# The last 384 tokens leave the sort: a plain store in place of an indirect scatter for the MLP's last step

## What is computed

```python
skip_score = x @ w_skip
do_compute = skip_score > 0
out = x.copy()
xc = x[do_compute]
e_idx = np.argmax(xc @ w_gate, axis=1)
for e in range(E):
    mask = e_idx == e
    h = np.maximum(xc[mask] @ w1[e], 0.0)
    y[mask] = gate_w[mask, None] * (h @ w2[e])
out[do_compute] = xc + y                 # skipped tokens keep x
# the MLP, on all 2304 tokens
h = out @ w_in
return np.maximum(0.01 * h, h) @ w_out
```

## Time and profile before

| | us |
|---|---|
| median of 3 runs | 777.68 |
| lowest and highest run | 777.25, 777.89 |
| the profiled execution, its own time | 777.04 |
| its span, from the first to the last instruction | 775.0 |
| TensorE matmul busy | 715.4 (92%) |
| VectorE, ScalarE, GpSimd busy | 276.1, 262.1, 183.9 |

### The profile page before, as it was taken

The page is one execution under the profiler, slowest core; times in us unless marked ns, Lnnn a source line. Parts: engine busy times, 40 slices in busy tenths (PEclk is TensorE's granted clock), DMA queues, the critical chain, the costliest instruction groups (busy, mean ns, idle before and its releaser), DMA issues.

```text
span 775.0 us, 12847 instructions
## 1 busy us (share of the span) xinstructions
PE 715.4 (92%) x4627; PEld 663.4 (86%) x4627; DVE 276.1 (36%) x577; ACT 262.1 (34%) x522; POOL 183.9 (24%) x185
## 2 busy tenths in 40 slices
PE   2989989991999999998999999999999999999994
PEld 2888878871999999997898999999998989899993
DVE  4667757757000000004323242333224333323221
ACT  4687776550111221113222222222222232223221
POOL 2120100103786667533000500230050013001001
PEclk9999999995899999999999999999999999999997
DMA  8483745788799999953000300120030012001001
GB/s 175 111 185 99 189 125 168 235 266 197 221 316 329 316 301 315 328 167 100 1 1 1 122 1 1 41 82 1 0 120 1 0 41 81 0 0 41 1 1 41
DMA packets 72920, 91.46 MB, mean 118 GB/s; under 512 B 26704, under 2 KB 47728, under 8 KB 72881
## 3 DMA queue, kind: packets, MB, share of 16 engines
q1 hardware_dynamic: 63537, 65.35, 29.5%
q0 software_dynamic: 8288, 25.57, 11.6%
q10 hardware_dynamic: 1056, 0.02, 0.1%
HBM read 73.91 MB, written 17.01 MB: 117 GB/s over the span
## 4 chain that ended last, share of the span: by engine, by line
PE 79%; SPq 6%; ACT 4%; DVE 4%; issue 3%; DMA 3%; another core or an unknown queue 2%; POOLq 0%; POOL 0%; ACTq 0%; DVEq 0%
PE psum L1568 26%; PE psum L1587 26%; PE psum L1481 9%; PE psum L1497 8%; SPq L395 4%; ACT kt L784 2%; PE psum L1321 2%; PE psum L1346 1%; DMA wg<-in_moe_w_skip_dram 1%; PE psum L1419 1%; SPq L380 1%; PE psum L1436 1%; PE psum L1507 1%; PE psum L1299 1%
## 5 line engine op out<-in xcount | busy, mean ns | idle before, releaser
L1568 PE MATMUL psum<-x2h,wih 128*128 128x384 f32 x384 | 130.6, 340 | 1.9 <-DVE x2l L1241 1.9
L1259 DVE SCALAR_TENSOR_TENSOR g_act<-g_raw 128x384 f32<-128x384 f32 x96 | 53.6, 558 | 219.3 <-ACT g_raw L947 205.5
L1568 PE MATMUL psum<-x2h,wil 128*128 128x384 f32 x384 | 129.5, 337 | 0.0
L1568 PE MATMUL psum<-x2l,wih 128*128 128x384 f32 x384 | 129.0, 336 | 0.0
L947 ACT ACTIVATE g_raw<-psum 128x384 f32<-128x384 f32 x96 | 47.2, 492 | 235.2 <-PE psum L1568 226.9
L1587 PE MATMUL psum<-woh,g_l 128*128 128x512 f32 x288 | 114.0, 396 | 0.0
L1587 PE MATMUL psum<-wol,g_h 128*128 128x512 f32 x288 | 113.7, 395 | 0.0
L1587 PE MATMUL psum<-woh,g_h 128*128 128x512 f32 x288 | 112.1, 389 | 0.7 <-DVE g_l L1263 0.7
L745 POOL DMA_INDIRECT out_dram<-o_sb,idxo x18 | 18.9, 1050 | 337.8 <-ACT o_sb L942 334.1
L1481 PE MATMUL psum<-xt,wring 128*128 128x160 f32 x512 | 81.2, 306 | 0.7 <-ACT xt L873 0.6
L1497 PE MATMUL psum<-hp,wring 128*128 128x160 f32 x512 | 77.4, 299 | 0.0
(11 more groups left out here) (173 smaller groups left out, 896.0 us busy)
## 6 DMA issues: line engine op xcount, KB each, us to landing
wring<-in_moe_w_dram SPq DMA_DIRECT2D x64, 512.0 KB, 8.5
y_rows<-zrow SPq DMA_DIRECT2D x1, 4800.0 KB
q_st<-in_q_dram SPq DMA_DIRECT2D x8, 576.0 KB
k_st<-in_k_dram SPq DMA_DIRECT2D x8, 576.0 KB
x_sb<-x_rows SPq DMA_DIRECT2D x4, 1024.0 KB, 5.9
stage<-in_moe_w_in_dram POOLq DMA_DIRECT2D x4, 1024.0 KB, 8.4
stage<-in_moe_w_out_dram POOLq DMA_DIRECT2D x4, 1024.0 KB, 9.8
vs<-in_v_dram SPq DMA_DIRECT2D x20, 128.0 KB, 7.0
```

What stands on the lines that cost most here:

```text
L1259: dve.scalar_tensor_tensor(out=g_act[:, f % 2, :], in0=g_raw[:, f % 2, :], scalar=LEAK, in1=g_raw[:, f % 2, :], op0=ALU.mult, op1=ALU.max) ...
L1568: last = pe.matmul(bank[f % 2][:, 0:MT * P], wt[:, c, f * P:(f + 1) * P], xp[:, T.par, c, :], start=(c == 0 and n == 0), stop=(c == KD - 1 ...
```

## The change

`HEAD` = `NT` - `MT` = 15 blocks, that is 1920 tokens, are put in order. The last 384 tokens keep their places: their entries of `pos_i` are written as constants by GpSimd (an iota). Ranks are computed for the head alone, and the class totals come from a new matmul `COUNTS` over the head's 15 blocks and a VectorE sum `cnt`. The last step's rows are then contiguous in `out`, and SyncE stores them with three plain DMAs from `o_sb`; GpSimd's last `scatter_out` is gone. The record scatters and the gathers of the last step stay indirect.

```diff
@@ setup
+    HEAD = NT - MT
+    out_tok = out.rearrange("(t p) n -> p t n", p=P)
@@ sync
             y_store(last_tile)
-            sp.wait_ge(s_out, 16 * MT * NM)
+            for j in range(MT):
+                if j == 1:
+                    sp.wait_ge(s_ov, NM)
+                else:
+                    sp.wait_ge(s_oa, 2 * NM - 1 + j // 2)
+                sp.dma_start(out_tok[:, HEAD + j, :], o_sb[:, j, :]).then_inc(s_oh, 16)
+            sp.wait_ge(s_out, 16 * MT * (NM - 1))
+            sp.wait_ge(s_oh, 16 * MT)
             sp.wait_ge(s_zd, 32)
             sp.wait_ge(s_sct, 16 * NT)
@@ gpsimd
             step(pool.memset(rec[:, :, 3], 0))
+            step(pool.iota(pos_i[:, HEAD:NT], pattern=[[P, MT]], base=P * HEAD, channel_multiplier=1))
...
-            scatter_out(NM - 1)
@@ vector
-            step(dve.tensor_scalar(planf[:, 29:30], RANKS[0:1, NT, 0:1], float(MT * P), None, ALU.is_lt))
+            dve.wait_ge(s_ct, 1)
+            step(dve.reduce_sum(cnt[:, :], COUNTS.rearrange("p t e -> p e t"), AX.X))
+            step(dve.tensor_scalar(planf[:, 29:30], cnt[0:1, 0:1], float(MT * P), None, ALU.is_lt))
...
-            C3 = [P, NT, E + 1]
-            step(dve.tensor_tensor(cbp[:, :, :], free(RANKS[:, NT, :], [P, E + 1, E + 1], 1),
+            C3 = [P, HEAD, E + 1]
+            step(dve.tensor_tensor(cbp[:, :, :], free(cnt[:, :], [P, E + 1, E + 1], 1),
                                    c_tril[:, :, :], ALU.mult))
...
-            step(dve.tensor_tensor(posc[:, :, :], RANKS[:, 0:NT, :], free(cb[:, :], C3, 1), ALU.add))
-            step(dve.tensor_tensor(posc[:, :, :], posc[:, :, :], ohb[:, 0:NT, :], ALU.mult))
+            step(dve.tensor_tensor(posc[:, :, :], RANKS[:, 0:HEAD, :], free(cb[:, :], C3, 1), ALU.add))
+            step(dve.tensor_tensor(posc[:, :, :], posc[:, :, :], ohb[:, 0:HEAD, :], ALU.mult))
             step(dve.reduce_sum(pos[:, :], posc[:, :, :], AX.X))
-            dve.tensor_copy(pos_i[:, :], pos[:, :]).then_inc(s_rec, 1)
+            dve.tensor_copy(pos_i[:, 0:HEAD], pos[:, :]).then_inc(s_rec, 1)
@@ tensor
             last.then_inc(s_rk, 1)
+            pe.matmul(COUNTS, onesb[:, :], ohb[:, 0:HEAD, :], start=True, stop=True).then_inc(s_ct, 1)
@@ constants
-POOL_ALL = 29
+POOL_ALL = 30
```

More of the change, by code:

```diff
@@ L165, in attention_experts_mlp @@
     cb = at(r, "cb", [P, E + 1])
-    posc = at(r, "posc", [P, NT, E + 1])
-    pos = at(r, "pos", [P, NT])
+    cnt = at(r, "cnt", [P, E + 1])
+    posc = at(r, "posc", [P, HEAD, E + 1])
+    pos = at(r, "pos", [P, HEAD])
     c_base = at(r, "c_base", [P, E])
@@ L270, in attention_experts_mlp @@
         s_rec = sem("s_rec")
+        s_ct = sem("s_ct")
+        s_oh = sem("s_oh")
         s_sct = sem("s_sct")
@@ L307, in attention_experts_mlp @@
         RANK = RANKS[:, :, 1:E + 1]
+        COUNTS = bank[5][:, 0:HEAD * (E + 1)].rearrange("p (t e) -> p t e", e=E + 1)
         Y = psum[:, 4 * 512:8 * 512].rearrange("d (c t) -> d c t", c=KD)
```

## The result

| | before | changed |
|---|---|---|
| median | 777.89 us (5 runs) | 773.70 us (5 runs) |
| lowest and highest | 777.25, 780.22 | 772.05, 777.40 |
| the profiled execution | 777.04 | 777.40 |
| its span | 775.0 | 775.2 |

The ratio of changed to before is 0.9926, with a 95% interval of 0.9898 to 0.9954: faster by 5.8 us, between 3.6 and 7.9. The medians lie 4.2 us apart, a ratio of 0.9946, which the interval holds. The measurement with the changed kernel was repeated twice, each time beside new runs of the kernel before, and gave 0.9912 (0.9885 to 0.9939) and 0.9940 (0.9922 to 0.9958).

A forecast was written before the change was run, and what follows sets the result against it. TensorE bounds the kernel, with matmuls for 715.4 of 775.0 us; only the 10.4 us after its last matmul could pay. Tail 5.3 us, the rest 0: 777.68 - 5.3 = 772.4, taken as 772.3, range 770.9 to 774.2.

The forecast's parts named there:

- A: Main forecast: scatter's issue and GpSimd's DRAIN both leave the end; 772.3 us (771.2 to 773.6), gain 4.6 to 5.9, chance 0.83.
- The tail: After the last matmul: SyncE's three plain stores replace GpSimd's scatters; span ends at 769.7 instead of 775.0, gaining 5.3 us.
- the rate: Traffic of the three last stores: 786 KB at 266 to 348 GB/s, taken as 2.7 us.
- the fast end: Last stores at 348 GB/s, seen with one output block alone in flight: 2.26 us of traffic, gain 5.9 us.
- The DRAIN: GpSimd's closing DRAIN, 7.577 us, ending at 774.7; forecast over by about 714, covered by 50 us of matmuls.
- rival B: At the end: 3.1 us of closing follow the last landing of any queue; gain 2.1, time 775.5 us, chance 0.10.
- Rival C: SyncE's last stores land one after another, 6.4 us each; slower, 787.7 us, chance 0.02.
- Rival D: First expert matmuls: TensorE's return to 2.4 GHz shifts, winning or losing up to half of 4.5 us; 770.0 or 774.6, chance 0.05.
- What was put at nothing: Edits ahead of the last matmul, in routing and token order: 0 us, routing plus or minus 0.3 us.
- The reduce in front of the `plan`: Routing stage, VectorE: one more reduce, up to 0.3 us, under 4.5 us of cover from the first gather.
- the end of the `pos` chain: Routing stage, VectorE: starts 0.3 us later, three steps a sixth shorter, so its end moves by 0.2 us at most.
- The test I had set: If the last matmul doesn't end at 764.6 within half a microsecond, something ahead of the tail was not free.

The follow-up runs named there:

- block signals: Changed kernel, with TensorE signalling each block of the last step, so each is copied and stored once done: 772.00 us, ratio 0.9926 against the kernel before.
- the late wait: Changed kernel, with GpSimd made to wait for the last copy to `o_sb` and run nothing behind it: 777.28 us in one run, no ratio.
- a late memset: Changed kernel, with GpSimd waiting for the last copy to `o_sb`, then running one small memset: 774.81 us, ratio 0.9946 against the kernel before.

## Why the prediction was right, point by point

**The size.** The forecast was 772.3 us, and 5.3 us of gain; measured were 773.7 and a ratio that stands for 5.8. The median lies 1.4 us above the forecast, inside the range but 0.1 above the 773.6 given for A, and that it came so near is in part luck: attention alone moves by 4.5 us, and the median of the kernel before was 777.9, 780.1 and 778.0 in three measurements. The gain is what was forecast; the absolute time hangs on those. The first profile shows attention 4 us longer in one of the five runs; that it was longer in the other runs above 773 too is likely, but they have no trace.

**The tail.** Every step that was named is in the trace. Counted from the last matmul, the first issue was put at 0.75 us and came at 0.66; the third at 1.65, and came at 1.6; traffic at 1.55, and came at 1.5. From the end of traffic to the end of the span 0.85 was allowed, and it took 0.9. The mis-sized term is the rate. The pair of stores after an expert tile ran at 266 GB/s, and I put 2.7 us for the 786 KB. The three blocks ran at 377 to 393 GB/s and took 2.1 to 2.2 us, below even the fast end given, 2.26. That accounts for the 0.5 us by which the gain was better. The sum for the fast end was itself off: 2.26 in place of 2.7 us makes a gain of 5.7, not 5.9. The pair has 80 rows in each store and the blocks 128; the difference may lie there, but no run varied it.

**The DRAIN.** It was right that it leaves the path, and the cover named for it, 50 us of matmuls, is there. I had charged it to the DMAs just issued, if only by weighing it in that way against rival B. The runs show something simpler: 4.8 us from GpSimd's last instruction, whatever it was, and 5.0 to 5.1 where it was a DMA. What a reader should take from the earlier trace rows is the 5.0 us to GpSimd's own last instruction, and not the 3.3 us to SyncE's landing, which is what is left of the 5.0 once the last transfer's own time is taken off.

**Rival B,** 3.1 us of closing behind the last landing of any queue, fell with the first trace: 0.2 us lay between SyncE's DRAIN and the end. **Rival C,** stores that land one after the other and lose from 3.05 us each, fell too: they landed 2.1 to 2.5 us after their issue, and overlapped. **Rival D,** the clock, did not cost what was put on it, but it does move. The stretch at 1.2 GHz that begins in the routing stage lasted 23.9 us in every trace, before and changed. Where it ends against the expert matmuls differs: these ran at 1.2 GHz for 4.5 us in before and for 3.8, 4.9 and 5.3 us in the three traces of the changed kernel, so at half the clock up to 0.4 us were won or lost. The extremes of the ten traces, 3.0 us with block signals and 6.1 with the scatter put back, belong to kernels with the same edits ahead of the tail, so an effect of the new matmul doesn't stand out. The window of the changed kernel's first profile:

```profile
202.00:205.80 3.80, 3.77 (x14) 3.80 (x15) 0.00 (x0) 0.30 (x1) 2.65 (x3) 0.50 0.34 108
```

**What was put at nothing.** The scatter put back shows all of it at once, 1.0000 with 0.2% to either side. The reduce in front of the `plan` cost 0.34 us (0.3 expected), hidden behind the first gather, and the end of the `pos` chain moved by 0.26 (0.2 at most expected), hidden as well. The test I had set, that the last matmul ends at 764.6 within half a microsecond, would have misled: it ended at 770.7, from a slower attention stage. A test on one absolute time can't tell a change from the scatter of a stage far ahead of it; the length of each stage can.

## What to carry to other kernels

Look at which engine's closing DRAIN ends last, and move the last work off an engine whose DRAIN is long: here three stores on SyncE, in place of GpSimd, took 5.8 us off a program of 778, of which 3.4 came from the queue and 2.4 from the form of the DMA. To read a tail, measure it from the last matmul to the end of the span and compare stage by stage; whole spans differed by 5 us between executions of the same kernel. When the end of a kernel is a store, let each piece go as soon as it is done: the three blocks needed 2.1 us of traffic in one store or in three, so what can be moved is when the first of it starts. With block signals the tail fell to 3.3 us.

## What the runs showed of the hardware that I had not expected

GpSimd's DRAIN at the end of a program took 4.81 us when nothing ran ahead of it (in the five traces in which its last DMA was long past, and with the late wait), 4.93 around a late memset, and ended 5.0 to 5.1 us after the last DMA issued by GpSimd. SyncE's took 0.013 us each time. The DRAINs of TensorE, VectorE and ScalarE ended within 0.1 us of their own last instruction; in the changed kernel ScalarE's ran from 770.8 to 771.9, and its last copy ended at 771.8.

Three plain DMAs issued by GpSimd took 1.70 us, where three indirect ones took 3.55 (766.11 to 769.66 in before).

Up to its last matmul the MLP stage has the same work for TensorE in all kernels. It took 409.6 to 409.9 us in seven of the ten traces, but 411.0 to 411.4 in three, one of them of the changed kernel. In those three, and in no other, TensorE was granted the lower level, 1.2 GHz, for 3.4 us shortly after the stage began; at half the clock that is worth up to 1.7 us. It had waited 1.9 us for the first MLP inputs in all ten, so the wait alone doesn't decide it. The window of that stretch in the second repeat of the changed kernel:

```profile
355.70:359.10 3.40, 3.40 (x12) 3.40 (x11) 0.00 (x0) 0.00 (x0) 1.98 (x4) 0.50 0.10 20
```
